# Where the experts' weight buffers lie in SBUF, when their loads start, and who splits the first weights

## The chip, the cores and the metric

One core of a Trainium2 chip runs the whole program. The metric is the device time of one execution in microseconds.

## The reference

Three stages follow each other on B x S = 4 x 768 = 3072 tokens. First a delta-rule attention over 8 heads of 48, whose outputs make x, 3072 x 384. Then a dense block, and at last eight experts of which each token takes all, weighted:

```python
h = x @ w_in                                   # 384 -> 2048
g = h * np.tanh(np.log1p(np.exp(h)))           # (h kept where h > 20)
x = g @ w_out                                  # 2048 -> 384

logits = x @ w_gate                            # 384 -> 8
P = np.exp(logits - logits.max())
for _ in range(8):                             # rows, then columns
    P /= P.sum(1, keepdims=True) + 1e-09
    P /= P.sum(0, keepdims=True) + 1e-09
    P *= N / E
for e in range(E):                             # 8 experts, 384 -> 1024 -> 384
    out += P[:, e:e + 1] * (np.maximum(x @ w1[e], 0.0) @ w2[e])
```

All is float32.

## The kernel before

The attention phase (the first 520 us or so) is not touched. It leaves x transposed in SBUF as two tensors of one 32-bit format for TensorE, x_hi and x_lo, whose sum is x: [128, 3, 3072] each, 36864 bytes of a partition. They are the first two tensors of SBUF, one behind the other.

**Products in three parts.** Every float32 product is three matmuls of 128 x 128 weights with 512 moving columns: high weights with high data, high weights with low data, low weights with high data (`three`). TensorE loads the weights of the next matmul while one runs (PEld).

**Dense phase** (`dense_programs`). Six blocks of 512 tokens (tb), in each 16 steps f. A step multiplies x by the weights of 128 hidden units (9 matmuls into h_bank[f % 4], "up") and, three steps behind, the result g of step f - 3 by w_out (9 matmuls into three y banks, "down"). Between them, ScalarE and VectorE turn h into g_hi and g_lo: VectorE's product of line 770 (`de_hg<-de_hg,de_rec`) and its difference of line 750 (`de_g_lo`) read two SBUF tensors each. The finished block replaces x in x_hi and x_lo. The first and the last block are written out, the others are a loop. `h_read(f)` and `w2_read(f)` are the semaphore and the count that say that the last block's up (down) matmuls of steps below f are done, so that their weights may be overwritten. `prepare(f)` is what an engine does extra at step f of the last block.

**Gate.** 36 matmuls (6 blocks x 3 parts m of the model dimension x high and low of x) with 16 columns of weights: `gate[:, m]` holds the high and the low part of w_gate for part m, 64 bytes of a partition for each m.

**Experts.** 8 experts x 2 halves g of the hidden units x 6 blocks tb, each with 4 up groups j of 9 matmuls (`ex_h`) and 4 down groups of 9 (`ex_y`), two behind. ScalarE takes relu of h_bank[j] into r_hi (`hi_ready`), VectorE makes r_lo (`lo_ready`), and adds y, weighted by the rows of P in pb, into acc. The first and the last expert are written out, the six between are a loop.

Weights of a half (1.5 MB) come by one DMA of the SP queue into `stage`, and are split while the other half is in use: ScalarE copies a sixth of stage to w[g][0] (line 1032, at the end of each step tb), GpSimd subtracts it from stage into w[g][1] (line 1001). SP starts the next load when all six pieces are split (`wlo_ready`). Before each step tb SP also loads pb from p_rows. The weights of the first half are split inside the last dense block: ScalarE's pieces in steps f = 10 to 15, by `prepare`.

**Memory.** gate_in (96 bytes) and gate (192 bytes) lie behind x_lo, then one tensor "area", in which `at(name, offset, ...)` places all of the two phases by hand; the experts' buffers take the room of dense weights that are read. `half` is 12288 bytes, six times 2048, and all offsets of weights, r and g in the area are multiples of 2048. Weight tiles of 128 columns are 512 bytes long, so they start at multiples of 512 within their buffer:

```python
w = [[at("ex_w0_hi", 2 * half, ...), at("ex_w0_lo", 4 * half, ...)],
     [at("ex_w1_hi", half, ...), at("ex_w1_lo", 3 * half, ...)]]
```

## Time and profile before

| | |
|---|---|
| median of 3 runs | 2570.56 us (2567.76 to 2571.11) |
| the profiled execution | 2566.92 us, of which 2565.0 us from the first to the last instruction |
| mean granted clock of TensorE | 0.975 of full speed (2.4 GHz) |
| busy | TensorE 97%, its weight loads 81%, VectorE 51%, ScalarE 34%, GpSimd 17% |
| attention, dense, gate, experts | to about 520, 940, 948 and 2565 us |

Matmuls are pipelined: the trace gives one of 512 columns some 390 ns, while the next one starts 230 ns after it. The spacing is therefore read from starts, and the busy share says only that TensorE had work. "issue" is time in which an engine waited for nothing that the profile shows. Durations of neighbouring matmuls tell apart those that were held up a little from those that weren't.

### The profile page before, as it was taken

How to read it: one execution, taken by the hardware profiler on the slowest of the kernel's cores; microseconds unless marked ns; L12 is line 12 of the kernel's file. 1: busy time of each engine (PE TensorE's matmuls, PEld its weight loads, DVE VectorE, ACT ScalarE, POOL GpSimd, SP SyncE). 2: the span in 40 equal slices, each digit the busy share in tenths (PEclk: the TensorE clock that was granted, in tenths of full speed). 3: DMA queues.
4: the chain of work that ended last, by engine and by line, in shares of the span. 5: the costliest groups of instructions: out<-in, count | busy, mean ns of one | idle time of the engine just before them, and what ended most of it. 6: DMA issues, size and time to landing. Idle time of an engine off the chain costs nothing.

```text
span 2565.0 us, 39836 instructions
## 1 busy us (share of the span) xinstructions
PE 2487.6 (97%) x15288; PEld 2070.5 (81%) x15288; DVE 1297.4 (51%) x2426; ACT 875.6 (34%) x1900; POOL 430.6 (17%) x350
## 2 busy tenths in 40 slices
PE   6999989989999999999999999999999999999999
PEld 5888888878888868788878887887887887888887
DVE  5766557678777765443333333333333333333344
ACT  5867557756666641111111111111111111111111
POOL 7665547300000011100000000000000000000000
PEclk9989779989999999999999999999999999999999
DMA  1110101020000010110101101101101011011013
GB/s 60 43 43 22 43 23 37 2 86 13 0 0 0 25 32 1 43 41 17 42 14 41 41 13 47 41 13 42 41 17 42 9 49 39 13 45 41 17 25 70
DMA packets 58883, 79.31 MB, mean 31 GB/s; under 512 B 37584, under 2 KB 38352, under 8 KB 56656
## 3 DMA queue, kind: packets, MB, share of 16 engines
q1 hardware_dynamic: 54256, 63.33, 8.1%
q10 hardware_dynamic: 4464, 13.50, 1.6%
q8 instruction: 139, 2.28, 0.4%
q14 instruction: 24, 0.20, 0.0%
HBM read 71.81 MB, written 5.01 MB: 30 GB/s over the span
## 4 chain that ended last, share of the span: by engine, by line
PE 76%; issue 2%; DVE 1%; ACT 0%; DMA 0%; POOL 0%; DVEq 0%; ACTq 0%; POOLq 0%
PE ex_h L52 38%; PE ex_y L52 37%; DVE de_hg L770 0%; DVE de_en L757 0%; DVE de_g_lo L750 0%; DMA de_stage<-w_in 0%; ACT de_g_hi L703 0%; DVE de_en L755 0%; DVE de_w_lo L739 0%; POOL ex_w_lo L1001 0%; DVE ex_term L1116 0%; DVE ex_acc L1130 0%; PE ex_logits L52 0%; POOL ex_col L1017 0%; ACT de_en L709 0%
## 5 line engine op out<-in xcount | busy, mean ns | idle before, releaser
L1162 DVE SCALAR_TENSOR_TENSOR ex_r_lo<-ex_h,ex_r_hi 128x512 fp32r<-128x512 f32 x384 | 264.5, 690 | 963.6 <-ACT ex_r_hi L1050 963.6
L1050 ACT ACTIVATE ex_r_hi<-ex_h 128x512 fp32r<-128x512 f32 x384 | 229.5, 598 | 1334.1 <-PE ex_h L52 1334.1
L52 PE MATMUL ex_h<-x_lo,ex_w_hi 128*128 128x512 f32 x1152 | 456.8, 397 | 12.3 <-issue 12.3
L52 PE MATMUL ex_h<-x_hi,ex_w_hi 128*128 128x512 f32 x1152 | 456.6, 396 | 0.0
L52 PE MATMUL ex_h<-x_hi,ex_w_lo 128*128 128x512 f32 x1152 | 456.1, 396 | 0.0
L52 PE MATMUL ex_y<-ex_r_hi,ex_w_hi 128*128 128x512 f32 x1152 | 451.3, 392 | 1.2 <-DVE ex_r_lo L1162 1.2
L52 PE MATMUL ex_y<-ex_r_lo,ex_w_hi 128*128 128x512 f32 x1152 | 449.0, 390 | 0.0
L52 PE MATMUL ex_y<-ex_r_hi,ex_w_lo 128*128 128x512 f32 x1152 | 448.8, 390 | 0.0
L1001 POOL TENSOR_TENSOR ex_w_lo<-ex_stage,ex_w_hi 128x512 fp32r<-128x512 f32 x96 | 124.4, 1295 | 1748.8 <-ACT ex_w_hi L1032 1714.0
L52 PEld LDWEIGHTS ex_h<-x_hi,ex_w_lo 128*128 128x128 f32 x1152 | 216.8, 188 | 65.9 <-issue 13.3
L52 PEld LDWEIGHTS ex_h<-x_hi,ex_w_hi 128*128 128x128 f32 x1152 | 216.5, 188 | 50.6 <-issue 0.5
L52 PEld LDWEIGHTS ex_y<-ex_r_hi,ex_w_hi 128*128 128x128 f32 x1152 | 217.0, 188 | 49.5 <-DVE ex_r_lo L1162 1.6
L52 PEld LDWEIGHTS ex_h<-x_lo,ex_w_hi 128*128 128x128 f32 x1152 | 216.5, 188 | 49.9
L52 PEld LDWEIGHTS ex_y<-ex_r_lo,ex_w_hi 128*128 128x128 f32 x1152 | 216.8, 188 | 47.3
L52 PEld LDWEIGHTS ex_y<-ex_r_hi,ex_w_lo 128*128 128x128 f32 x1152 | 216.7, 188 | 47.2
L1116 DVE TENSOR_TENSOR ex_term<-ex_y,ex_pb 128x512 f32<-128x512 f32 x255 | 159.7, 681 | 2.1 <-PE ex_y L52 2.1
L1130 DVE TENSOR_TENSOR ex_acc<-ex_acc,ex_term 128x512 f32<-128x512 f32 x255 | 160.5, 685 | 0.1
L52 PE MATMUL ex_h<-x_hi,de_w_hi 128*128 (+1 forms) x288 | 114.9, 399 | 8.1 <-DVE de_w_lo L739 8.1
L52 PE MATMUL ex_y<-de_g_hi,de_w_hi 128*128 128x512 f32 x288 | 113.6, 395 | 5.7 <-DVE de_g_lo L750 5.7
L52 PE MATMUL ex_h<-x_lo,de_w_hi 128*128 (+1 forms) x288 | 114.6, 398 | 0.0
L52 PE MATMUL ex_h<-x_hi,de_w_lo 128*128 (+1 forms) x288 | 114.3, 397 | 0.0
L52 PE MATMUL ex_y<-de_g_lo,de_w_hi 128*128 128x512 f32 x288 | 112.8, 392 | 0.0
(135 smaller groups left out, 3346.9 us busy)
## 6 DMA issues: line engine op xcount, KB each, us to landing
ex_stage<-w_exp SPq DMA_DIRECT2D x16, 1536.0 KB, 6.3
ex_pb<-p_rows SPq DMA_DIRECT2D x90, 256.0 KB, 3.3
at_qT<-q_t ACTq DMA_DIRECT2D x10, 512.0 KB, 4.6
at_v_in<-v ACTq DMA_DIRECT2D x11, 384.0 KB, 3.2
at_k_in<-k ACTq DMA_DIRECT2D x10, 384.0 KB, 4.9
out<-ex_stage SPq DMA_DIRECT2D x60, 64.0 KB, 2.0
de_stage<-w_in SPq DMA_DIRECT2D x8, 384.0 KB, 3.3
de_stage<-w_out SPq DMA_DIRECT2D x8, 384.0 KB, 3.2
```

The costliest lines, as they stand in the source:

```text
L52: return nc.tensor.matmul(out, lhsT, rhs, start=start, stop=stop)
L1001: nc.gpsimd.tensor_tensor(w[g][1][:, cols], stage[:, cols], w[g][0][:, cols].bitcast(F32), ALU.subtract).then_inc(wlo_ready, 1)
L1050: nc.scalar.activation(r[0][:, j, :], h_bank[j][:], ACT.Relu).then_inc(hi_ready, 1)
L1116: nc.vector.tensor_tensor(t, y, p, ALU.mult).then_inc(term_ready, 1)
L1130: nc.vector.tensor_tensor(a, a, t, ALU.add).then_inc(acc_ready, 1)
L1162: nc.vector.scalar_tensor_tensor(out=r[1][:, j, :], in0=h_bank[j][:], scalar=0.0, in1=r[0][:, j, :].bitcast(F32), op0=ALU.max, op1=ALU.sub ...
```

## The change

1. gate_in and gate are allocated behind the area instead of ahead of it. The area thereby begins where x_lo ends.
2. Inside the area the experts' buffers move: w0_hi by 64 bytes, w1_hi by 16 (a tensor of four more columns, of which the first four are not used), w1_lo by 128, w0_lo by 256, and all behind them (term, pb, r, out_last and the small ones) by 512. The dense phase's tensors and stage keep their place in the area. Since w0_hi and w0_lo now reach a few bytes into the ninth step's dense weights, their writers wait for one step more: `h_read` and `w2_read` of DF // 2 + 1.
3. SP's load of the next weights waits, besides for the last split, for the second relu of the new half (`hi_ready`). The load of pb stands behind it in SP's program.
4. The first half's weights are split by GpSimd alone: for each of six pieces a copy stage to w0_hi and the subtraction, after the first load has landed and the ninth down step of the last dense block is done. ScalarE's six copies inside `prepare` go.

```diff
@@ -845,12 +845,12 @@
         s, sd = Scope(nc, ctx, "ex"), Scope(nc, ctx, "de")
         p_rows = nc.dram_tensor("p_rows", (E, N), F32, kind="Internal").ap()
         lg_rows = nc.dram_tensor("lg_rows", (2 * E, N), F32, kind="Internal").ap()
-        gate_in = s.sb("gate_in", [P, MC * E])
-        gate = s.sb("gate", [P, MC, 2, E], F32R)
         half = DF // 2 * DM * 4
         AREA = 8 * half + 8 * 2 * DM + 16 * 4 * TB + 32
         base = nc.sbuf_base
         s.sb("area", [P, AREA // 4])
+        gate_in = s.sb("gate_in", [P, MC * E])
+        gate = s.sb("gate", [P, MC, 2, E], F32R)
 
         def at(name, offset, shape, dt=F32):
             size = 4
@@ -861,13 +861,21 @@
 
         assert half == 4 * 2 * GW
         stage = at("ex_stage", 0, [P, 2 * GW])
-        w = [[at("ex_w0_hi", 2 * half, [P, 2 * GW], F32R), at("ex_w0_lo", 4 * half, [P, 2 * GW], F32R)],
-             [at("ex_w1_hi", half, [P, 2 * GW], F32R), at("ex_w1_lo", 3 * half, [P, 2 * GW], F32R)]]
-        term = at("ex_term", 5 * half, [P, MC, TB])
-        pb = at("ex_pb", 5 * half + 4 * MC * TB, [P, RB, TB])
-        r = [at(f"ex_r_{n}", 6 * half + 4 * i * FC * TB, [P, FC, TB], F32R) for i, n in enumerate(("hi", "lo"))]
-        out_last = at("ex_out_last", 6 * half, [P, TC, DM])
-        small = 6 * half + 8 * FC * TB
+        skew = {"w1_hi": 0, "w0_hi": 64, "w1_lo": 128, "w0_lo": 256, "rest": 512}
+
+        def weights(name, offset, head):
+
+            t = at("ex_" + name, offset + skew[name], [P, head + 2 * GW], F32R)
+            return t[:, head:head + 2 * GW]
+
+        w = [[weights("w0_hi", 2 * half, 0), weights("w0_lo", 4 * half, 0)],
+             [weights("w1_hi", half, 4), weights("w1_lo", 3 * half, 0)]]
+        rest = skew["rest"]
+        term = at("ex_term", 5 * half + rest, [P, MC, TB])
+        pb = at("ex_pb", 5 * half + rest + 4 * MC * TB, [P, RB, TB])
+        r = [at(f"ex_r_{n}", 6 * half + rest + 4 * i * FC * TB, [P, FC, TB], F32R) for i, n in enumerate(("hi", "lo"))]
+        out_last = at("ex_out_last", 6 * half + rest, [P, TC, DM])
+        small = 6 * half + rest + 8 * FC * TB
         ident = at("ex_ident", small, [P, P])
         prob = at("ex_prob", small + 4 * P, [P, E, NT])
         lg = at("ex_lg", small + 4 * (P + E * NT), [P, 2 * E, NT])
@@ -942,7 +950,7 @@
         def _(sp):
             dense.sp(sp)
             sp.dma_start(gate_in[:], w_gate).then_inc(gate_loaded, 16)
-            sp.wait_ge(*dense.h_read(DF // 2))
+            sp.wait_ge(*dense.h_read(DF // 2 + 1))
             sp.dma_start(stage[:], w_exp[0, 0]).then_inc(staged0, 16)
             sp.wait_ge(gated_ready, NB)
             sp.dma_start(lg_rows, logitsT).then_inc(lg_stored, 16)
@@ -970,6 +978,7 @@
                 if tb == 0 and not last_group(e, g):
 
                     sp.wait_ge(wlo_ready, (2 * e + g + 1) * PIECES)
+                    sp.wait_ge(hi_ready, steps_before(e, g, 0) * FC + 2)
                     sp.dma_start(stage[:], w_exp[e + g, 1 - g]).then_inc(staged, 16)
                 if first(e) and g == 0:
                     return
@@ -1002,8 +1011,11 @@
                                         ALU.subtract).then_inc(wlo_ready, 1)
 
             dense.pool(pool)
-            pool.wait_ge(*dense.w2_read(DF // 2))
+            pool.wait_ge(staged0, 16)
+            pool.wait_ge(*dense.w2_read(DF // 2 + 1))
             for i in range(PIECES):
+                cols = slice(i * PW, (i + 1) * PW)
+                nc.gpsimd.tensor_copy(w[0][0][:, cols], stage[:, cols]).then_inc(whi_ready, 1)
                 split(0, 0, i)
 
             def step(e, g, tb):
@@ -1023,10 +1035,7 @@
         @block.scalar
         def _(act):
             def split(e, g, i):
-                if first(e) and g == 0:
-                    if i == 0:
-                        act.wait_ge(staged0, 16)
-                elif i == 0:
+                if i == 0:
                     act.wait_ge(staged, 16 * (2 * e + g))
                 cols = slice(i * PW, (i + 1) * PW)
                 nc.scalar.copy(w[g][0][:, cols], stage[:, cols]).then_inc(whi_ready, 1)
@@ -1035,8 +1044,6 @@
                 if f == 0:
                     act.wait_ge(gate_loaded, 16)
                     nc.scalar.copy(gate[:, :, 0, :], gate_in[:].rearrange("p (m e) -> p m e", m=MC)).then_inc(ghi_ready, 1)
-                if f >= DF - PIECES:
-                    split(0, 0, f - DF + PIECES)
 
             dense.act(act, prepare)
```

## Rows read from the trace of the kernel before

**Rows 1.** The page: busy time, the chain's shares by line, issue to landing.
```profile
PE 2487.6 (97%) x15288; PEld 2070.5 (81%) x15288; DVE 1297.4 (51%) x2426; ACT 875.6 (34%) x1900; POOL 430.6 (17%) x350
...
PE ex_h L52 38%; PE ex_y L52 37%; DVE de_hg L770 0%; DVE de_en L757 0%; DVE de_g_lo L750 0%; DMA de_stage<-w_in 0%; ACT de_g_hi L703 0%; DVE de_en L755 0%; DVE de_w_lo L739 0%; POOL ex_w_lo L1001 0%; DVE ex_term L1116 0%; DVE ex_acc L1130 0%; PE ex_logits L52 0%; POOL ex_col L1017 0%; ACT de_en L709 0%
...
ex_stage<-w_exp SPq DMA_DIRECT2D x16, 1536.0 KB, 6.3
```

**Rows 2.** Windows: busy us (instructions) of each engine, then clock, DMA share, GB/s.
```profile
1560.00:1740.00 180.00, 180.00 (x783) 146.73 (x782) 66.54 (x107) 31.91 (x55) 14.20 (x11) 1.00 0.08 24
...
560.00:860.00 300.00, 300.00 (x1303) 244.04 (x1302) 236.47 (x385) 188.53 (x312) 0.00 (x0) 1.00 0.03 9
```

**Rows 3.** The chain in the experts, 1300 to 1600 us: start, length, what.
```profile
1302.30 2.10 PE ex_h L52 x9
...
1339.62 2.10 PE ex_h L52 x9
```

**Rows 4.** The chain in the experts, 1555 to 1575 us.
```profile
1556.19 2.04 PE ex_y L52 x9
1558.23 2.10 PE ex_h L52 x9
```

**Rows 5.** The chain in the dense phase, from 889 us.
```profile
889.86 2.10 PE ex_h L52 x9
891.96 2.04 PE ex_y L52 x9
```

**Rows 6.** TensorE's groups by operands, 1560 to 1740 us: busy, mean ns.
```profile
L52 PE MATMUL ex_h<-x_lo,ex_w_hi 128*128 128x512 f32 x130 | 51.5, 396 | 0.0
...
L52 PE MATMUL ex_y<-ex_r_lo,ex_w_hi 128*128 128x512 f32 x131 | 51.0, 389 | 0.0
```

**Rows 7.** Timeline of TensorE in the gate: first to fourth of six.
```profile
945.37 0.39 PE L52 MATMUL ex_h<-x_hi,ex_gate 128*16 128x512 f32 x1
945.59 0.40 PE L52 MATMUL ex_h<-x_lo,ex_gate 128*16 128x512 f32 x1
945.83 0.40 PE L52 MATMUL ex_h<-x_hi,ex_gate 128*16 128x512 f32 x1
946.06 0.39 PE L52 MATMUL ex_h<-x_lo,ex_gate 128*16 128x512 f32 x1
```

**Rows 8.** Timeline of VectorE in the last dense block.
```profile
902.87 0.68 DVE L770 TENSOR_TENSOR de_hg<-de_hg,de_rec 128x512 f32<-128x512 f32 x1
...
911.21 1.73 DVE L770 TENSOR_TENSOR de_hg<-de_hg,de_rec 128x512 f32<-128x512 f32 x1
...
930.90 1.65 DVE L770 TENSOR_TENSOR de_hg<-de_hg,de_rec 128x512 f32<-128x512 f32 x1
```

**Rows 9.** Timeline of TensorE at the dense phase's end, releasers in brackets.
```profile
929.15 0.50 PE L52 MATMUL ex_y<-de_g_hi,de_w_hi 128*128 128x512 f32 x1 [1.98 <-DVE de_g_lo L750]
...
934.04 0.53 PE L52 MATMUL ex_y<-de_g_hi,de_w_hi 128*128 128x512 f32 x1 [2.53 <-DVE de_g_lo L750]
...
934.79 0.63 PE L52 MATMUL ex_y<-de_g_hi,de_w_lo 128*128 128x512 f32 x1
935.22 0.63 PE L52 MATMUL ex_y<-de_g_hi,de_w_hi 128*128 128x512 f32 x1
```

**Rows 10.** GpSimd's groups over the span.
```profile
L1001 POOL TENSOR_TENSOR ex_w_lo<-ex_stage,ex_w_hi 128x512 fp32r<-128x512 f32 x96 | 124.4, 1295 | 1748.8 <-ACT ex_w_hi L1032 1714.0 <-issue 34.9
```

**Rows 11.** Timeline of the SP queue at a loop edge.
```profile
1344.42 0.33 SPq L973 DMA_DIRECT2D ex_stage<-w_exp  x1
```

**Rows 12.** Timeline of ScalarE behind that loop edge.
```profile
1354.52 0.60 ACT L1050 ACTIVATE ex_r_hi<-ex_h 128x512 fp32r<-128x512 f32 x1 [4.11 <-PE ex_h L52]
...
1363.33 0.61 ACT L1032 CAST ex_w_hi<-ex_stage 128x512 fp32r<-128x512 f32 x1
```

**Rows 13.** The chain at the next loop edge, 1535 to 1560 us.
```profile
1547.53 2.48 issue
```

**Rows 14.** TensorE's waits: in total, times, longest.
```profile
PE ex_h L52 <- issue: 12.3, 5, 2.7
```

## The prediction

> **What bounds the kernel.** First the page. TensorE is busy for 97% of the span, and the chain that ended last is TensorE in the experts for 75% of it, halved between ex_h (up) and ex_y (down) [rows 1]. The reader should take from this that the other engines matter only where they hold TensorE up. Then the stages: in the quiet stretches TensorE is busy all the time at the full granted clock, 783 matmuls in 180.00 us and 1303 in 300.00 us, 230 ns from one to the next in both phases [rows 2]. So the kernel's time is the number of matmuls times their spacing, plus a few holes. In the experts there are 8 x 2 x 6 x 4 = 384 pairs of nine up and nine down matmuls, in the dense phase 6 x 16 = 96 pairs.
>
> The chain of waits prices a pair: nine pairs take 1339.62 - 1302.30 = 37.32 us, 4.147 us each [rows 3]. The halves are unequal: nine up take 2.10 us, nine down 2.04, in the experts [rows 4] as in the dense phase, where they make 4.14 [rows 5], although both stream 512 columns over 128 x 128 weights. Averages by operand say the same: up matmuls last 396 ns, down ones 389 [rows 6]. Something costs the up matmuls about 7 ns each, and it lies where the change works.
>
> **Where the 7 ns come from.** x_hi and x_lo fill 36864 bytes each, 18 x 2048, so every moving tile of x starts on one grid. Before the change 96 bytes of gate_in and 192 of gate follow, so all that lies in "area" is 288 bytes off that grid: weights, r, g alike. A down matmul moves r or g while the next weights are loaded from the same area: difference 0 (modulo 512, the size of a weight tile; all offsets of tiles inside a buffer are multiples of it). An up matmul moves x beside weights at +288. I read this as a cost that hangs on the offset between the moving tile and the weights that are loaded beside it. The gate matmuls test it, since they move x beside weights at 96, 160 and 224 (96 + 64m). Two of each six last 0.40 us and the others 0.39 [rows 7]: the second (its neighbour load is m = 1, offset 160) and the third (offset 160 again); those beside offsets 224 and 96 are the short ones. 160 and 288 are both 32 modulo 128; 0, 96 and 224 are 0 or 96. So the trace has one costly residue, 32, and two free ones. That x itself is not slow to stream is seen in the same rows.
>
> A rule of the Trainium skill speaks against this (SBUF — State Buffer, "Who interferes with whom", and TensorE: Matmul & The Clock Gate on LDWEIGHTS): TensorE has two independent read ports, and loading the next weights takes nothing from the matmul that runs. By it the offsets are worth 0 us. The 396 against 389 ns don't agree with it, at least not for every offset [rows 6].
>
> **The change, part by part.**
>
> *Gate buffers last.* The area moves to offset 0. In the dense phase weights, g and x are all on the grid: difference 0 up and down, the free residue. A pair should take 2 x 2.04 = 4.08 instead of 4.147 us: 0.067 us. DVE and ACT must follow: in the stretch where GpSimd holds DVE up, a step takes (930.90 - 911.21) / 4 = 4.92 us, of which about 1.0 is the wait (1.73 and 1.65 against 0.68) [rows 8], so their own cycle is 3.92 us and fits under 4.08. About 7 of the 96 pairs lie where DVE, not TensorE, sets the pace. 89 x 0.067 = 6.0 us gained.
>
> *The skew.* Moving tiles are then at 0 (x) and 512 (r), both 0. Weights: w0_hi 64, w0_lo 256 = 0 mod 128, w1_hi 16, w1_lo 128 = 0 mod 128. Of three loads two are of hi and one of lo. The lo loads get the free residue. For 16 and 64 the trace has no row. Bounds: fast as 0 and 96 are, or slow as 32 is; a slow load costs 0.067 us / 9 = 7.4 ns, since nine of them lie beside the nine up matmuls of a pair. Both fast: 384 x 0.067 = 25.7 us gained. A half of the groups (g = 0 has w0, g = 1 has w1) with hi loads that cost pays 12 x 7.4 = 89 ns a pair against the present 67, so it loses 192 x 0.022 = 4.2 us, and with free ones it wins 12.8. 64 is as near to 96 as to 32, 16 as near to 0 as to 32. I take both as fast, because three of four known places are (0, 96 and 96 again at 224, against 32), and keep the other end.
>
> *First split by GpSimd.* Gone: six ACT casts of 0.6 us and their pacing. Added: six GpSimd copies, 128 x 512. Nearest rows: GpSimd's subtraction of two inputs of that size takes 1.295 us, ACT's cast of it 0.61 [rows 10, 12]. The copy lies between; I take 1.0. Now every GpSimd operation meets the DVE product of line 770 and holds it for 1 us, five times, because ACT releases GpSimd just then; TensorE pays at the drain, with waits of 1.98 and 2.53 us [rows 9]. These exist in part without GpSimd: with no more steps to fill, down(14) and down(15) wait for the elementwise chain. Afterwards twelve operations follow each other without pacing from down(8) on, 6 x 1.29 + 6 x 1.0 = 13.7 us of reads. The upper bound is that DVE stands for all of it but its idle time: in 3.5 steps, 3.5 x (4.15 - 3.27) = 3.1 us idle (DVE is busy 236.47 of 300 us [rows 2], 3.27 us of a pair) and 3.5 x 0.68 = 2.4 us in the product that reads PSUM, so 8.2 us of delay against 5 x (4.92 - 4.15) = 3.9 now: +4.3 us, +5 with some matmuls at the low clock. The lower bound is that DVE slips in between and the present 3.9 us go, and the low clock that follows with them. It ends before the last steps, so some is caught up, and ACT is freed of 3.6 us: I take 0. Here the Trainium skill (SBUF — State Buffer, the shared port pair) says that a GpSimd operation that reads SBUF and a DVE one with two SBUF inputs block each other whole; the trace agrees, 0.68 us alone against 1.65 beside GpSimd [rows 8]. Who waits behind: the first up matmul of the experts wants half of the low parts, but the 36 gate matmuls, 36 x 0.23 = 8 us, come first. Hidden.
>
> *Weight loads later.* SP now also waits for the second relu of the group. At a loop edge it issues the load at 1344.42 [rows 11]; the second relu starts at 1354.52 and lasts 0.60 [rows 12]; the load takes 6.3 us to land [rows 1], so it is there at about 1361.6. ACT wants it at 1363.33 [rows 12]: 1.7 us to spare. Were that cover gone, ACT would stand at the cast and the next relu with it, which has some 4 us of idle time before it (4.11 [rows 12]). Queued behind it on SP are the p_rows copies; the first is wanted by DVE a whole step (16.6 us) later. Cost 0. What could it bring? TensorE stands 2.48 us in "issue" one matmul after a loop edge [rows 13], 12.3 us in five such holes [rows 14]. SP issues the load about then. But the hole opens before its data move, and "issue" is time in which TensorE waits for nothing that the profile shows, no weight of this load among it. I take 0; the bound is 1 us of each hole, 5 us, and one or two spells of the low clock behind a hole. A spell costs 2 us: at the lower level of the granted clock, 1.2 GHz, matmuls start 0.43 us apart instead of 0.23 [rows 9], and I put ten of them to a spell.
>
> **Sum.** The profiled execution took 2566.92 us: 2565.0 of span and 1.9 around it; it is 3.6 us under the median of 2570.56. 2566.92 - 6.0 - 25.7 = 2535.2; on the median, 2538.9. Forecast 2539 us, 1.2% faster.
>
> **Rivals.**
> - *One of the two new offsets is slow.* Gain 6.0 + 12.8 - 4.2 = 14.6: 2556. For: 32 is slow and both adjoin it. Chance 0.20; with a milder price per load it lies between this and the forecast.
> - *Both slow.* -6.0 + 2 x 4.2 = +2.4 us: 2573. For: as above, twice. Chance 0.07.
> - *The address does nothing.* Two reads of TensorE don't disturb each other, and up and down differ for another reason (nine matmuls into one bank against three). Only the dense tail moves, 2570.56 - 4 to + 5: 2567 to 2575. Against: the gate matmuls [rows 7] differ in little but the address of the load. Chance 0.07. This is what the rule of the Trainium skill on the two ports (SBUF — State Buffer) would give.
> - *Slower: it is the moving tile's own start that counts.* x starts at a multiple of 64 bytes, r and g at 32 more; the first is slow and the second fast. Afterwards r and g start like x, and every down nine takes 2.10: (384 + 96) x 0.06 = +28.8 us: 2599. Against it: the gate matmuls move x and most are short. It decides as soon as the added cost of a down nine passes 10 ns (5.1 us over 480). Chance 0.12, which also takes in smaller losses in which the new offsets cost more than 32 does.
> - *Deeper gain.* 512 columns at 2.4 GHz are 213 ns and the fast spacing is 2.04 / 9 = 227: if 16 and 64 also remove part of that, say 5 ns at each of the 4608 loads of hi in the experts, it is 23 us more: 2516. No row shows any spacing below 227 for such matmuls. Chance 0.08. The Trainium skill gives N / 2.4 + 2.5 ns back to back (TensorE: Matmul & The Clock Gate), an estimate of 216 ns here; no stretch of this trace reaches it.
> - *The forecast*, both fast: 0.46, with its own range of 2533 to 2546.
>
> "Same" is within 0.2%, 5.1 us, about what a measurement can tell here. Faster: 0.46 + 0.20 + 0.08 = 0.74, less 0.02 where the dense tail eats a gain. Same: those 0.02 and 0.10 of the 0.14 of "both slow" and "nothing". Slower: 0.12 and the other 0.04. The range runs from 2531 to 2573: below it lies the deeper gain, above it the moving tile's start and the worst of the rest.
>
> **What the profile afterwards would show.** In the chain, nines of 2.04 both up and down in both phases, and 4.08 us a pair. If only g = 0 or g = 1 keeps 2.10, that half's offset (64 or 16) is slow, and down nines there rise too. If down nines go to 2.10 in the dense phase as well, the moving tile's start counts. If up nines stay at 2.10 in the dense phase, where all differences are 0, the reading by offsets is wrong altogether. The gate matmuls will lie at 0, 64 and 128 from x: long ones beside m = 1 would show 64 slow. GpSimd should show twelve operations in a row after about 910 us, and the two waits at the drain about as long as now; loop edges as now. The prediction is wrong if 16 or 64 has a price of its own, or if DVE loses more than a few microseconds to the twelve.

## The result, and the profile after

The changed kernel takes 2583.83 us (median of seven executions, 2578.44 to 2594.35), the kernel before 2570.56 (seven, 2565.34 to 2577.34). The ratio is 1.0054 [1.0034, 1.0075]: 0.5% slower, where 2539 us and 1.2% faster were forecast. The profiled execution took 2586.76 us, with a span of 2584.6 and a mean granted clock of 0.973.

The table sets the stages of the profiled executions beside each other, in us from the start of the span: the first matmul of each stage, and the end.

```
                 dense     gate   experts       end    dense    experts
before          531.65   939.86    948.12   2565.04    408.2     1616.9
after           537.52   941.26    949.60   2584.64    403.7     1635.0
```

The dense phase gained 4.5 us and the experts lost 18.1, +13.6 together; the medians differ by 13.3. That this execution reaches the dense phase 5.9 us later is an attention phase that the change doesn't touch.

The page of the changed kernel, lines that answer to [rows 1]: TensorE has the same share, and the chain is TensorE in the experts as before.

```profile
PE 2504.1 (97%) x15288; PEld 2078.2 (80%) x15288; DVE 1296.8 (50%) x2426; ACT 871.3 (34%) x1894; POOL 435.9 (17%) x356
...
PE ex_h L52 37%; PE ex_y L52 36%; DVE de_en L757 1%; DVE de_hg L770 1%; DVE de_g_lo L750 1%; DVE de_w_lo L739 1%; DVE de_en L755 0%; ACT de_g_hi L703 0%; DMA de_stage<-w_in 0%; POOL ex_w_lo L1010 0%; DVE ex_term L1123 0%; DVE ex_acc L1137 0%; DVE de_hg L764 0%; ACT de_en L709 0%; PE ex_logits L52 0%
...
ex_stage<-w_exp SPq DMA_DIRECT2D x16, 1536.0 KB, 6.5
```

Nothing here tells the two kernels apart. The windows do, read as in [rows 2] (both in the changed kernel): 1320 matmuls in the dense stretch instead of 1303, but 774 in the experts' instead of 783. TensorE is busy and at the full granted clock in both.

```profile
1560.00:1740.00 180.00, 180.00 (x774) 145.46 (x773) 67.89 (x109) 30.71 (x54) 12.83 (x10) 1.00 0.11 36
560.00:860.00 300.00, 299.61 (x1320) 247.29 (x1319) 240.36 (x392) 191.12 (x317) 0.00 (x0) 1.00 0.04 11
```

The chain of the changed kernel says which half changed. In the experts (answering to [rows 4]) the down nines went from 2.04 to 2.10 us, and the up nines stayed at 2.10:

```profile
1571.46 2.10 PE ex_y L52 x9
1573.56 2.10 PE ex_h L52 x9
```

In the dense phase (to [rows 5]) the up nines went to 2.04:

```profile
850.49 2.04 PE ex_h L52 x9
852.53 2.04 PE ex_y L52 x9
```

So the dense phase did what was forecast of it, and the experts the opposite. The groups of the changed kernel by operands show that the down matmuls of all three kinds last longer, not those beside one kind of load alone (in the kernel before, in the same window, 391, 389 and 389; the last is in [rows 6]):

```profile
L52 PE MATMUL ex_y<-ex_r_hi,ex_w_hi 128*128 128x512 f32 x129 | 51.4, 398 | 0.0
L52 PE MATMUL ex_y<-ex_r_hi,ex_w_lo 128*128 128x512 f32 x129 | 51.1, 396 | 0.0
...
L52 PE MATMUL ex_y<-ex_r_lo,ex_w_hi 128*128 128x512 f32 x129 | 50.7, 393 | 0.0
```

The chain rounds to 0.01 us. Below, nines are therefore sums of the mean distances between starts over all experts, in ns. A nine at 226.7 ns from start to start is 2040 ns and is called free; at 233.3 ns it is 2100 and is called costly.

```
             w0_hi w0_lo w1_hi w1_lo  r    g=0 up  down    g=1 up  down
before, to x   288   288   288   288 288   2100.7 2046.0   2100.8 2046.8
after           64   256    16   128   0   2101.2 2098.4   2096.3 2095.1
```

(Bytes modulo 512, from x_hi's grid.) A pair is 4.20 us in g = 0 and 4.19 in g = 1, against 4.147. (4.1955 - 4.147) x 384 = +18.6 us, and 408.2 to 403.7 in the dense phase: that is the whole result. Both g = 0 and g = 1 are costly throughout a product, although the prediction had the lo loads at 128 and 256 free. The means of g = 1 hide one half that differs: in expert 0 its nines are 2068 and 2065 on average, against 2098 to 2101 in the other seven experts, at the same placement. It begins at 2100 and runs at 2060 (228.9 ns a matmul) from 1068 us on, behind a wait of TensorE of 0.74 us. So one placement can run at more than one spacing; the last experiments take this up.

### The profile page after: what moved, and what is told of

It reads as the page before. It is cut to its first block, busy times and chain, and to the rows that moved or that the text cites. A ratio compares the mean times of both kernels' runs of the same rounds, so it can differ in the third digit from the quotient of the medians.

```text
span 2584.6 us, 39851 instructions
## 1 busy us (share of the span) xinstructions
PE 2504.1 (97%) x15288; PEld 2078.2 (80%) x15288; DVE 1296.8 (50%) x2426; ACT 871.3 (34%) x1894; POOL 435.9 (17%) x356
## 4 chain that ended last, share of the span: by engine, by line
PE 73%; DVE 3%; issue 2%; ACT 0%; DMA 0%; POOL 0%; DVEq 0%; ACTq 0%; POOLq 0%
PE ex_h L52 37%; PE ex_y L52 36%; DVE de_en L757 1%; DVE de_hg L770 1%; DVE de_g_lo L750 1%; DVE de_w_lo L739 1%; DVE de_en L755 0%; ACT de_g_hi L703 0%; DMA de_stage<-w_in 0%; POOL ex_w_lo L1010 0%; DVE ex_term L1123 0%; DVE ex_acc L1137 0%; DVE de_hg L764 0%; ACT de_en L709 0%; PE ex_logits L52 0%
## 5 line engine op out<-in xcount | busy, mean ns | idle before, releaser
L52 PE MATMUL ex_y<-ex_r_hi,ex_w_hi 128*128 128x512 f32 x1152 | 458.2, 398 | 0.7 <-DVE ex_r_lo L1169 0.7
L52 PE MATMUL ex_y<-ex_r_hi,ex_w_lo 128*128 128x512 f32 x1152 | 455.6, 395 | 0.0
L52 PE MATMUL ex_y<-de_g_hi,de_w_lo 128*128 128x512 f32 x288 | 112.3, 390 | 0.0
```

The lines of the kernel that those rows point to most:

```text
L52: return nc.tensor.matmul(out, lhsT, rhs, start=start, stop=stop)
```

## The experiments

Two theories stood at first. **A**, the prediction's, mended: the distance modulo 128 counts, and 64 and 16 are costly for a whole product. **B**: the two reads of TensorE don't care about addresses; the later load or GpSimd's split slow the experts down.

### Undoing parts: grid_all, gate_last, times_only

grid_all is the changed kernel with all of the area on one grid:

```diff
-        skew = {"w1_hi": 0, "w0_hi": 64, "w1_lo": 128, "w0_lo": 256, "rest": 512}
+        skew = {"w1_hi": 0, "w0_hi": 0, "w1_lo": 0, "w0_lo": 0, "rest": 0}
...
-             [weights("w1_hi", half, 4), weights("w1_lo", 3 * half, 0)]]
+             [weights("w1_hi", half, 0), weights("w1_lo", 3 * half, 0)]]
```

> The changed kernel with all five skews at 0, so that x, r, g and all weights start on one grid; the split by GpSimd and the later loads stay. By offsets (the cost hangs on the distance between the moving tile and the weights loaded beside it, and 0 is free): nines of 2.04 us up and down in both phases, 4.08 us a pair, and against the kernel before 384 x 0.067 + 6 = 31 us less, about 2540 us. If the skews were harmless and the split or the later loads cost the time, it stays near the changed kernel's 2584 us and the nines in the experts stay at 2.10.

gate_last is the kernel before with the two gate buffers behind the area and nothing else:

```diff
-        gate_in = s.sb("gate_in", [P, MC * E])
-        gate = s.sb("gate", [P, MC, 2, E], F32R)
...
         s.sb("area", [P, AREA // 4])
+        gate_in = s.sb("gate_in", [P, MC * E])
+        gate = s.sb("gate", [P, MC, 2, E], F32R)
```

> The kernel before with nothing but gate_in and gate moved behind the area. By offsets: the same 4.08 us a pair, about 31 us less than before, 2540 us; the difference from the kernel with all skews at 0 is then the price of the split by GpSimd together with the later loads, which I put between -4 and +5 us. If the address does nothing: 2570 us as before.

times_only is the changed kernel with the gate buffers ahead of the area again and all skews 0, so that what stays of the change are the later loads, the waits of one step more and GpSimd's split.

> The kernel before, its placement untouched, with the split by GpSimd, the later loads and the two waits of one step more. By offsets: pairs of 4.147 us as before and within 5 us of 2570 us, since only the end of the dense phase moves. If the split or the later loads are what makes the changed kernel slower: +13 us, 2584.

Measured against executions of the kernel before that were made beside them (median 2567.37 us): grid_all 2542.86 us, ratio 0.9896 [0.9875, 0.9918]; gate_last 2542.32, 0.9891 [0.9872, 0.991]; times_only 2570.26, 1.0003 [0.9991, 1.0014]. The chain of grid_all in the experts has both halves free:

```profile
1570.95 2.04 PE ex_h L52 x9
1572.99 2.04 PE ex_y L52 x9
```

and that of times_only has the halves of the kernel before:

```profile
1571.37 2.04 PE ex_y L52 x9
1573.42 2.10 PE ex_h L52 x9
```

B falls: the new times of loads and splits cost nothing that this measures, and the experts' loss comes and goes with the placement alone. grid_all and gate_last also bear out the forecast's idea of distance 0: they gain 24.5 and 25.1 us where "all free" was reckoned at 31.7. And they settle the rival that up and down nines differ by their banks (nine matmuls into one against three): in gate_last the banks are as before, and both nines take 2040 ns. So the change is a good part (the gate buffers, -1.1%), a neutral part and a bad one (the skews, +41 us on top of grid_all).

### The offsets by themselves: sweep

A program with none of the reference's work: 48 matmuls per placement, 512 columns over 128 x 128 weights, one after the other with no wait, x at byte 0 and the weights of all three loads at the offset named. (All four sweeps are single executions.)

```diff
+                    at = ws[i % 3] // 4 + 128 * (i % 12)
+                    mo = m // 4 + 512 * ((i // 2) % 3)
+                    last = nc.tensor.matmul(banks[i // 9 % 4][:], wt[:, at:at + 128], mv[:, mo:mo + 512],
```

> None of the reference's work: 48 matmuls each of 512 columns over 128 x 128 weights for every placement of weights and moving tile, in order: weights at 0, 16, 32 ... 496 bytes beside a moving tile at 0, then 4 and 8, then both shifted alike by 16, 32, 64, 128, 256, then the moving tile alone shifted by these, then triples of weights as in the experts with the third at another place. If the relative offset decides: 227 ns from start to start at 0, about 234 ns at 32, 160 and 288, 227 ns at 96 and 224, and 227 ns wherever both are shifted alike. If only residue 32 modulo 128 costs, 16 and 64 are free; by the changed kernel's trace they should cost 7 ns or more. If what costs is that high and low weights lie at different places, all sweeps with equal weights stay at 227 ns and only the last triples rise.

Measured: mean distance of starts in ns, the first twelve of each block left out. The value for 0 is that of the last block, since the first one has 427 ns from start to start in its first matmuls.

```
weights at   0 226.7   16 226.7   32 233.3   48 233.3   64 233.3   80 232.0
            96 234.4  112 233.3  128 233.3  144 233.4  160 233.4  176 230.0
           192 229.0  208 233.3  224 233.3  240 226.7  256 226.7  272 226.7
           288 233.3; 304 to 496 repeat 48 to 240
             4 232.4    8 230.7
both at     16 233.3   32 226.7   64 226.7  128 226.7  256 226.7
loads of a product in turn (hi, hi, lo):
(64,64,256) 233.4  (16,16,128) 233.4  (0,0,128) 231.0  (0,0,64) 231.1  (0,0,256) 226.7
```

The period is 256 bytes, not 128. 128 is costly in this run, 96 and 224 too, and 64. Free in it are 0, 16 and 240 modulo 256. But the blocks follow each other without a break, and sweep4 will show that a block can inherit its value (144, 233.4 here, is 226.7 there behind a free block). Entered from free matmuls and costly all the same are 4, 32, 288, (64,64,256) and (0,0,64) here, 64 in sweep4, (0,0,32), (0,0,160) and (0,128,256) in sweep3, and a lo load at 128 in hi0. For 96, 224 and (16,16,128), and for 128 in all three loads, no run shows it. The two triples of the change are both costly throughout, (64, 64, 256) although one load of three is at a free place. The row "both at" says that what counts is the distance between weights and moving tile, as long as both start at a multiple of 32. Both at 16 have distance 0 and are costly here, but behind a costly block; of equal starts off a multiple of 32 only "both at 48" in sweep2 is entered from a free block, and it costs, 230.0.

### The lo loads: lo256, hi0, by256

lo256 is the changed kernel with w1_lo at 256 in place of 128. If 16 is free, as the sweep has it, g = 1 should become free.

```diff
+        skew = {"w1_hi": 0, "w0_hi": 64, "w1_lo": 256, "w0_lo": 256, "rest": 512}
```

> The changed kernel with w1_lo at 256 instead of 128; the rest as changed (w1_hi 16, w0_hi 64, w0_lo 256). If a placement is free when each load lies within 16 bytes of a multiple of 256 from the moving tile: the g = 1 half goes to 2.04 us a nine, 4.08 a pair, and 192 pairs save 0.111 us each: 21 us less than the changed kernel, about 2562 us; the g = 0 half stays at 2.10. If it is high and low lying at different places that costs: both halves stay and so does the time, 2584 us.

hi0 is the changed kernel with both hi buffers at 0 and the lo ones left at 256 (g = 0) and 128 (g = 1).

```diff
+        skew = {"w1_hi": 0, "w0_hi": 0, "w1_lo": 128, "w0_lo": 256, "rest": 512}
```

> The changed kernel with both hi tensors at 0 (w1_lo stays 128, w0_lo 256). By the multiple of 256: g = 0 free (2.04 us a nine), g = 1 at 231 ns a matmul or 2.08 us a nine, as the sweep had for two loads at 0 and one at 128; 23 + 6 us less than the changed kernel, about 2555 us. If a load at 128 were free, as the prediction had it, g = 1 would be free as well: 2540 us. If different places for high and low cost: no gain in either half.

by256 has the four weight buffers and the rest at five different multiples of 256, off the 2 KB grid as the change has them.

```diff
+        skew = {"w1_hi": 0, "w0_hi": 256, "w1_lo": 512, "w0_lo": 768, "rest": 1024}
```

> The changed kernel with skews of 0, 256, 512 and 768 bytes and 1024 for the rest: off a 2 KB grid, and all four different, but all multiples of 256. By the multiple of 256: 2.04 us a nine everywhere, 44 us less than the changed kernel, about 2540 us. If it is the 2 KB grid that matters, or being different: 2570 us or more.

Measured: by256 2540.53 us, 0.9887 [0.9868, 0.9907], all nines 2040: buffers need not share a 2 KB grid, multiples of 256 do as well. hi0 2561.13 (2555 were expected), 0.9966 [0.9953, 0.998]: g = 0 is free (2040.3, 2040.0), g = 1 has 2080.0 and 2080.2, 231.1 ns a matmul, as the sweep had for (0, 0, 128). The two halves of one expert, in the chain of hi0:

```profile
1574.27 2.04 PE ex_h L52 x9
1576.31 2.04 PE ex_y L52 x9
...
1699.79 2.08 PE ex_y L52 x9
1701.87 2.08 PE ex_h L52 x9
```

So a lo load at 128 costs by itself, and one at 256 doesn't: 192 x 0.080 = 15.4 us more than grid_all by the nines, 18 by the medians. lo256 is a miss: 2583.29, 1.0059 [1.0036, 1.0082], where g = 1 at (16, 16, 256) was to be free; it has 2100.3 and 2099.5. A place that is free in the sweep is costly in the kernel. (g = 0, whose placement lo256 leaves alone, moved from 2101.2 to 2090.2. By expert it has two values, the down nines too: its up nines take 2100 in experts 0, 2, 4 and 5, and 2081 in 1, 3, 6 and 7. What chooses between them isn't explained.)

### Short loads, starts and the order of placements: sweep2

Again no work of the reference. The gate's matmuls load 16 columns, and the prediction read its residues from them; here the width of the load changes too.

```diff
+cases = [(0, (0,) * 3, c) for c in (128, 16, 32, 64, 96)]
+cases += [(0, (96,) * 3, c) for c in (16, 32, 64, 96)]
```

> Again none of the reference's work, 48 matmuls for every case: first weights of 128, 16, 32, 64 and 96 columns at 0, then 16, 32, 64 and 96 columns at 96, 224, 32 and 160 bytes from the moving tile; then triples (16,16,0), (16,16,256), (16,16,240), (0,0,16), (64,64,64), (128,0,0), (0,256,512), (0,0,32); then moving tile and weights both shifted by 4, 8, 16, 24, 32, 48, 96, 160; then the moving tile at 32 with weights at 16, 48 and 288; then weights at 12, 20, 24, 28, 1024 and 1280. If the gate misled because its loads are short: 16 columns at 96 and 224 are free (227 ns) and 128 columns at the same places are not (234, 233), with the step between them somewhere on the way; 16 columns at 32 and 160 cost. Triples of places that are free alone are free. Shifted alike, multiples of 32 are free and 4, 8, 16, 24, 48 are not.

Measured, in ns from start to start:

```
columns loaded     16     32     64     96
weights at 0    231.2  231.7  229.9  230.1
          32    231.2  230.0  231.9  228.9
          96    229.8  230.4  231.4  230.8
         224    231.1  233.3  230.8  226.7
128 columns: (0,256,512) 226.7  (64,64,64) 233.3  (16,16,256) 233.4  (0,0,16) 232.2
both at 32 226.7, 96 226.7, 160 226.7; 4 237.4, 16 233.4, 48 230.0
x at 32: weights at 288 226.7, at 48 233.4
1024 226.7  1280 226.7
```

With 16 columns no place is free: 0 costs 231.2, 96 229.8, 160 231.7. The expectation that 96 and 224 are free for 16 columns is missed. The gate's rows could not tell the places of 128-column loads apart. And (16, 16, 256) is 233.4 here, while 16 and 256 alone were 226.7 in the first sweep: something besides the placement decides at 16.

### Placement in the kernel: same_place, r32; loads that differ: sweep3

same_place puts lo and hi of a half at the same residue modulo 256, 64 in g = 0 and 16 in g = 1.

```diff
+        skew = {"w1_hi": 0, "w0_hi": 64, "w1_lo": 256, "w0_lo": 320, "rest": 512}
...
+             [weights("w1_hi", half, 4), weights("w1_lo", 3 * half, 4)]]
```

> The changed kernel with high and low weights of a half at the same place modulo 256: w0_hi 64 and w0_lo 320, w1_hi 16 and w1_lo 272. If consecutive loads must keep one place modulo 256 and this place must be within 16 bytes of the moving tile's: g = 1 free (2.04 us a nine), g = 0 still 2.10, and (0.111 x 192) = 21 us less than the changed kernel, 2562 us. If it is only that high and low differ, both halves become free: 2540 us. If any place off the grid costs, none.

r32 has weights and x on the grid, and all that was behind them, r among it, 32 bytes off: grid_all with `"rest": 32`.

> All weights and x on the grid, and only r (with term, pb and the rest behind it) 32 bytes off it: the mirror image of the kernel before, where x is off from weights and r. If the distance between the moving tile and the loads beside it decides: up nines 2.04 us, down nines 2.10, 384 x 0.06 = 23 us more than with everything on the grid, about 2565 us. If up matmuls cost more for a reason of their own (nine into one bank), both nines stay at 2.04.

sweep3 (no work of the reference) runs products whose third load differs, (0, 0, b), and some pairs at 16 and 240.

```diff
+        cases += [(0, (0, 0, b)) for b in range(16, 257, 16)]
```

> None of the reference's work. Moving tile at 0, loads in triples: (0,0,b) for b from 16 to 256 in steps of 16; then (16,16,272), (16,16,528), (16,16,32), (16,16,496), (240,240,496), (240,240,0), (64,64,320), (64,64,192), (0,256,0), (0,128,256), (16,0,16), (16,16,16); then the moving tile at 32 with (32,32,32), (32,32,288), (32,32,0), (48,48,48). If loads must keep one place modulo 256: (0,0,b) is free only at 256, (16,16,272), (16,16,528), (240,240,496), (0,256,0) and 32 with (32,32,288) are free (227 ns), all other mixed ones are not, and 64 with 320 costs 233 because it is away from the moving tile.

Measured: same_place 2582.28 us, 1.0046 [1.0027, 1.0064], a miss: 2562 were expected with g = 1 free, and both halves are costly (2102.0 and 2098.3; 2096.4 and 2099.8). r32 2580.24, 1.0038 [1.0017, 1.0058]; its chain:

```profile
1570.34 2.10 PE ex_y L52 x9
1572.44 2.08 PE ex_h L52 x9
```

Down nines move r beside weights at distance -32: 2100.9, as in the sweep. Up nines move x beside weights at distance 0 and should be free, but have 2078.4. I read this as a recovery that takes some nine matmuls, which is argued and not shown. In sweep4 (below) a block at 0 behind one at 64 begins with 230, 231, 236, 228, 233, 231, 226 and 227 ns before it stays at 226.7, and the up nine of r32 has 234.1, 229.2, 230.9, 230.9, 235.2, 228.6, 232.1, 230.7 and 226.8. The miss of the expectation (2565) is of this size: 384 x 0.038 = 15 us. Against the reading stands the mirror image, the kernel before: there the free down nines behind costly up nines have 232.5 ns once and 226.7 from the second matmul on. Why the free rhythm is back after one matmul there and after eight here is open.

sweep3: only b = 16, 144 and 256 give 226.7, where 256 alone was expected; 32 gives 233.3, 128 231.0, the rest 231 to 233. (16, 16, 272) gives 226.7 and (16, 16, 32) 233.3; (240, 240, 496), again a single residue, 228.3.

### Which rhythm a placement is entered from: g1_at_16, sweep4

Left open were why 16 is free in a sweep and costly in a kernel. Call the spacing that a stream has settled in its rhythm. Theory **C**: 0 modulo 256 restores the free rhythm by itself, 16 only keeps whichever it finds, and in same_place and lo256 it found the costly one of g = 0. Rival **D**: 16 is costly in a kernel, by the moving tile's change from x to r or by the waits. g1_at_16 has g = 0 at 256 and 512, and g = 1 at 16 and 272, both buffers with four columns ahead:

```diff
+        skew = {"w1_hi": 0, "w0_hi": 256, "w1_lo": 256, "w0_lo": 512, "rest": 768}
...
+             [weights("w1_hi", half, 4), weights("w1_lo", 3 * half, 4)]]
```

> High and low weights of g = 0 on multiples of 256 (256, 512), those of g = 1 at 16 modulo 256 (16, 272), x and r at 0. If a spacing once free is kept at 16 and one that was disturbed is kept too: g = 1 enters from a free g = 0 at 2.04 us a nine and stays there until some wait disturbs it; the loop edges lie ahead of g = 0, which recovers by itself, so most of g = 1 is free and the time is near 2542 us. If 16 costs by its place: g = 1 at 2.10, 192 x 0.12 = 23 us more, 2565 us.

sweep4 (no work of the reference) runs each placement twice, once behind a block at 0 and once behind a block at 64:

```diff
+            for p in places:
+                cases += [free, p, costly, p]
```

> None of the reference's work. Each placement is run twice, once behind 48 matmuls with everything at 0 (227 ns) and once behind 48 with the weights at 64 (233 ns): weights at 0; 256; (0,256,512); 16; (16,16,272); (16,16,256); (0,0,16); (0,0,144); 240; moving tile and weights at 32; both at 96; weights at 144. If the rhythm is kept: multiples of 256 (and both shifted by 32 or 96) show 227 both times, 16 with its kin shows 227 behind the free block and 233 behind the costly one. If the place alone decides, both times are alike for each.

Measured: g1_at_16 2543.15 us, 0.9908 [0.9875, 0.9942]. The same g = 1 that had 2096 and 2100 in same_place is free in seven of eight experts (2039.5 to 2042.2). In sweep4:

```
                       behind 0   behind 64
0, 256, (0,256,512)       226.7       226.7
both at 32, both at 96    226.7       226.7
(16,16,256)               226.7       226.7
16, (16,16,272), 144      226.7       233.3
240                       226.7       228.4
(0,0,16)                  226.7       232.2
(0,0,144)                 226.7       232.5
```

Two windows of sweep4 show it in the trace's own terms; both lie in blocks with the weights at 16 (columns as in [rows 2], without ScalarE). Behind 0, 37 matmuls touch the 8 us, behind 64, 36, at the same granted clock:

```profile
156.00:164.00 8.00, 8.00 (x37) 6.64 (x36) 0.00 (x0) 0.00 (x0) 1.00 0.00 0
178.00:186.00 8.00, 8.00 (x36) 6.45 (x36) 0.00 (x0) 0.00 (x0) 1.00 0.00 0
```

C holds and D falls, for 16. lo256 isn't explained by it: (16, 16, 256) comes back to 226.7 in sweep4, but neither in sweep2 nor in that kernel. Nor are two rhythms enough: (64, 64, 256) has two costly ones in lo256, and (16, 16, 128) two in the changed kernel. The eighth expert's g = 1 (expert 0) is the other side of it. The timeline of TensorE in g1_at_16 shows the rhythm lost soon after that half begins, by durations as in [rows 7], and the chain then keeps it until g = 0 of the next expert. First the timeline:

```profile
1048.49 0.39 PE L52 MATMUL ex_y<-ex_r_hi,ex_w_hi 128*128 128x512 f32 x1
1048.72 0.40 PE L52 MATMUL ex_y<-ex_r_lo,ex_w_hi 128*128 128x512 f32 x1
1048.96 0.40 PE L52 MATMUL ex_y<-ex_r_hi,ex_w_lo 128*128 128x512 f32 x1
...
1059.26 0.50 PE L52 MATMUL ex_y<-ex_r_hi,ex_w_hi 128*128 128x512 f32 x1 [2.22 <-DVE ex_r_lo L1169]
```

and the chain of the same kernel behind the wait:

```profile
1067.38 2.10 PE ex_h L52 x9
1069.48 2.10 PE ex_y L52 x9
```

At 1048.72 TensorE isn't held up by anything that the trace shows; the wait of 2.22 us comes ten us later. What tipped it is not settled.

## Why the prediction was wrong

**What bounds the kernel, and the rows' 7 ns:** right. The time is the number of matmuls by their spacing; the offset between moving tile and loads sets it, as gate_last shows by moving two small buffers and nothing else, for 2567.37 - 2542.32 = 25 us between the medians. By the rule of the Trainium skill (SBUF — State Buffer, "Who interferes with whom"; TensorE: Matmul & The Clock Gate, "Step-by-step: what each phase is for", on LDWEIGHTS) loading the next weights takes nothing from the running matmul, and offsets would be worth nothing. The runs have 226.7 against 233.3 ns by the offset alone, so the measurement decides.

**The step that failed** is in "Where the 7 ns come from" and carried on in "The skew": "So the trace has one costly residue, 32, and two free ones", 0 and 96 modulo 128, and from it "w0_lo 256 = 0 mod 128" and "w1_lo 128 = 0 mod 128", "The lo loads get the free residue", and for 64 and 16 "I take both as fast, because three of four known places are". It put -25.7 us on the experts, which measured +18.1. Three things were wrong in it.
- The residues came from matmuls that load 16 columns. sweep2 shows that with such loads even 0 costs 231.2 ns and that the order of places isn't that of 128 columns. The one comparable row, the 0 of down nines, was right. In the changed kernel the gate's loads lie, by the sizes of what stands before them, at 128, 192 and 256 from x's grid, not at 0, 64 and 128 as the prediction had it. The timeline shows its matmuls alternating with the moving tensor, x_hi 0.40 and x_lo 0.39, and not with the place (against [rows 7]):

```profile
941.26 0.40 PE L52 MATMUL ex_logits<-x_hi,ex_gate 128*16 128x512 f32 x1
941.50 0.39 PE L52 MATMUL ex_logits<-x_lo,ex_gate 128*16 128x512 f32 x1
941.72 0.40 PE L52 MATMUL ex_logits<-x_hi,ex_gate 128*16 128x512 f32 x1
941.96 0.39 PE L52 MATMUL ex_logits<-x_lo,ex_gate 128*16 128x512 f32 x1
```

- The period is 256 bytes. A lo load at 128 costs by itself (hi0, g = 1: +40 ns a nine, not 0), and 64 costs behind a free block too (sweep4); 96 and 224 are costly in the sweep. 16 doesn't cost in itself (g1_at_16) but doesn't restore the free rhythm, and beside a lo load at 128 no run shows it free.
- A costly load was priced by itself, 7.4 ns each and 12 of 18 in a pair. In fact the price isn't added up load by load: (64, 64, 256), two costly loads of three, runs at 233.4 throughout, as (64, 64, 64) does, and (0, 0, 32) in sweep3, one of three, at 233.3; (0, 0, 128), also one of three, pays 4.4 ns a matmul on average. At 6.7 ns each a pair would pay 18 x 6.7 = 120 ns; measured are 4.1955 - 4.080 = 0.1155 us. So the rival "Both slow", the nearest to what happened, gave 2573 us and not 2584: 12 x 7.4 = 89 ns became 115.5, and 384 x 0.027 = +10.2 us.

**The moved start,** the rival for slower: x, r and g start at 0 modulo 32 in all kernels, r at x's grid is free in grid_all, and in the sweeps both at 32, 64 and 96 run at 226.7. It falls, although the down nines did rise as it said; its own test, the dense down nines, stayed at 2.04. "Deeper gain" falls too: no block of any sweep had a mean under 226.6 ns. The estimate of 216 ns that the prediction drew from the Trainium skill (TensorE: Matmul & The Clock Gate, "Back-to-back issue gap") was reached by no run.

**Gate buffers last:** right. 89 x 0.067 = 6.0 us reckoned, 4.5 measured in the dense phase with the split on GpSimd and, in gate_last without it, 408.2 - 402.2 = 6.0. In grid_all the experts gained 1616.9 - 1594.2 = 22.7 of the 25.7. Their nines gained (60.3 + 6.3) x 384 = 25.6 us, as reckoned; but the pauses, all distances above 260 ns less 227 each, add up to 18.7 us in the kernel before and to 21.5 in grid_all (22.9 in gate_last). The prediction put their growth at nothing. The one in expert 0, where TensorE waits for VectorE's ex_r_lo, grew by itself from 1.56 to 2.48 us from start to start: an engine that comes sooner waits longer.

**First split by GpSimd:** 403.7 - 402.2 = +1.5 us between the changed kernel and gate_last, within the bounds of -3.9 and +5 and close to the 0 taken; times_only has 0.3 us more than the kernel before in the dense phase. The timeline of GpSimd in the changed kernel: a copy is 0.61 us once and 1.07 after that, against 1.0 taken, and the twelve end at 926.46, ahead of the drain.

```profile
912.06 0.61 POOL L1018 CAST ex_w_hi<-ex_stage 128x512 fp32r<-128x512 f32 x1 [380.98 <-PE ex_y L52]
912.75 1.63 POOL L1010 TENSOR_TENSOR ex_w_lo<-ex_stage,ex_w_hi 128x512 fp32r<-128x512 f32 x1
914.33 1.07 POOL L1018 CAST ex_w_hi<-ex_stage 128x512 fp32r<-128x512 f32 x1
...
925.17 1.29 POOL L1010 TENSOR_TENSOR ex_w_lo<-ex_stage,ex_w_hi 128x512 fp32r<-128x512 f32 x1
```

VectorE's products meanwhile (its timeline, as in [rows 8]) lie 5.62 and 7.24 us apart, so 1.5 + 3.2 us above the 4.08 of a step, where the kernel before lost 5 x 0.77. GpSimd's row of operations holds up not only this product, as the prediction had it: in the same timeline the difference of line 750 takes 1.66 us instead of 0.69, the operation of line 757 1.67 instead of 0.69, and that of line 755, with one input, 0.83 instead of 0.42.

```profile
912.50 0.72 DVE L770 TENSOR_TENSOR de_hg<-de_hg,de_rec 128x512 f32<-128x512 f32 x1
...
918.12 1.65 DVE L770 TENSOR_TENSOR de_hg<-de_hg,de_rec 128x512 f32<-128x512 f32 x1
...
925.36 1.65 DVE L770 TENSOR_TENSOR de_hg<-de_hg,de_rec 128x512 f32<-128x512 f32 x1
```

TensorE's long waits at the end of the phase are about as long as foreseen, three with 5.03 us together instead of two with 4.51 (timeline of TensorE, against [rows 9]):

```profile
928.59 0.47 PE L52 MATMUL ex_y<-de_g_hi,de_w_hi 128*128 128x512 f32 x1 [1.94 <-DVE de_g_lo L750]
...
932.42 0.50 PE L52 MATMUL ex_y<-de_g_hi,de_w_hi 128*128 128x512 f32 x1 [1.51 <-DVE de_g_lo L750]
...
936.34 0.50 PE L52 MATMUL ex_y<-de_g_hi,de_w_hi 128*128 128x512 f32 x1 [1.58 <-DVE de_g_lo L750]
```

Here the trace agrees with the Trainium skill's rule on the shared port pair (SBUF — State Buffer, "Who interferes with whom"): the product takes 0.68 us alone, and 1.65 with GpSimd at work. Where the product starts first, at 912.50, it takes 0.72, and GpSimd's subtraction beside it 1.63 instead of 1.29.

**Weight loads later:** right at 0. At the loop edge of the changed kernel SP issues the load behind the second relu, and ScalarE has the data when it comes to the cast. The SP queue's timeline, then ScalarE's:

```profile
1359.49 0.33 SPq L982 DMA_DIRECT2D ex_stage<-w_exp  x1
```

```profile
1358.70 0.60 ACT L1057 ACTIVATE ex_r_hi<-ex_h 128x512 fp32r<-128x512 f32 x1 [3.59 <-PE ex_h L52]
...
1367.11 0.60 ACT L1057 ACTIVATE ex_r_hi<-ex_h 128x512 fp32r<-128x512 f32 x1 [3.60 <-PE ex_h L52]
1367.60 0.61 ACT L1041 CAST ex_w_hi<-ex_stage 128x512 fp32r<-128x512 f32 x1
```

The cast has no wait in brackets: it follows the relu at once, 1.6 us after the load's 6.5 are over. And the five holes at loop edges are as they were ([rows 14]: 12.3 us), so the load's issue had no part in them. TensorE's waits in the changed kernel:

```profile
PE ex_h L52 <- issue: 12.4, 5, 2.6
```

**Not settled:** what inside TensorE or the memory makes the 6.6 ns and remembers the rhythm (that it is tied to the placement is shown by runs, a mechanism is not); the values between, 228 to 232 ns; what chooses between two costly rhythms of one placement; why (16, 16, 256) is costly in lo256 and g = 0 changed there; why even the free distance is 226.7 and not 213; what tipped g = 1 of expert 0. The fastest versions measured, gate_last, grid_all and by256, are 1.0 to 1.1% faster than before, and their intervals overlap: the gate buffers' move alone has the whole gain.

## What to carry to other kernels

Where a stream of 512-column matmuls changes weights each time, as here, moving tiles and weights are best placed on the same residue modulo 256 bytes, and on multiples of 32: every such placement settled at 226.7 ns in the sweeps, and 0, 256, both at 32 and both at 96 did so behind a costly block too. A small buffer allocated ahead of them can cost 1% by its length alone. A rule on offsets has to be drawn from loads of the same width as those that it is used for, and measured with each placement entered from a free and from a costly stretch. One costly load in three is not a third of the price: at 32 bytes it held the whole stream at 233.3 ns, at 128 at 231.1. And where TensorE gets faster, part of the gain can go into waits that were partly hidden before (25.6 us of nines became 22.7).

## What the runs showed of the hardware that I had not expected

- The distance between starts takes 226.7 or 233.3 ns at most places (some settle between, at 228 to 232), with the period of 256 bytes in the distance from moving tile to weights, and the state is kept: weights at 16, (16, 16, 272) or 144 run at 226.7 behind a block at 0 and at 233.3 behind one at 64, for all 48 matmuls, while 0 and 256 come back to 226.7.
- Equal offsets are not enough: both at 32, 64, 96, 128, 160 and 256 give 226.7, but both at 48 230.0 behind a free block; both at 16 give 233.3 and both at 4 237.4, which were only entered from costly blocks.
- One placement can have two costly rhythms: (64, 64, 256) runs at 2100 or 2081 ns a nine by expert in lo256, (16, 16, 128) at 2100 or 2060 in the changed kernel.
- An operation of VectorE with one input (line 755) takes 0.83 us instead of 0.42 beside GpSimd's copies and subtractions.
- Loads of fewer columns are not cheaper: 16 columns at 0 give 231.2 ns, 128 columns 226.7.
- GpSimd copies 128 x 512 in 1.07 us, or 0.61 the first time.
